# Feature 128 of two neighbouring slices on two groups of 32 rows of the array, their two small products issued together

## The reference

```python
def _attn_ref(x):                       # x: 2 x 3008 x 256
    X = np.fft.fft(x, axis=1)
    X = np.fft.fft(X, axis=2)
    return X.real.astype(np.float32)

def _moe_ref(x, w_in, w_out):           # w_in 256 x 2048, w_out 2048 x 256
    h = x @ w_in
    g = np.where(h > 0.0, h, 1.0 * (np.exp(np.minimum(h, 0.0)) - 1.0))
    return (g @ w_out).astype(np.float32)

def _moe2_ref(x, w_in, w_out, alpha):   # the same shapes, alpha 2048
    h = x @ w_in
    g = np.maximum(h, 0.0) + alpha * np.minimum(h, 0.0)
    return (g @ w_out).astype(np.float32)
```

## Time and profile before

| | |
|---|---|
| median of 3 runs | 984.11 us (982.59 to 984.53) |
| the profiled execution's own time | 983.52 us |
| its span, first to last instruction | 981.7 us |
| outside the span | 1.8 us |
| TensorE busy (matmuls) | 964.7 us, 98%, 4466 matmuls |
| TensorE busy (weight loads) | 800.9 us, 82% |
| VectorE busy | 784.3 us, 80% |
| ScalarE busy | 621.1 us, 63% |
| GpSimd busy | 165.3 us, 17% |
| granted TensorE clock | 1.000 |

### The profile page before, as it was taken

One profiled execution on the slowest core, in us unless ns is written; L12 is line 12 of the kernel. 1 busy time (PEld: TensorE's weight loads), 2 busy tenths in 40 slices (PEclk: granted clock), 3 DMA queues, 4 the chain that ended last, 5 costly groups with the idle time before them and its releaser, 6 DMA issues.

```text
span 981.7 us, 12208 instructions
## 1 busy us (share of the span) xinstructions
PE 964.7 (98%) x4466; PEld 800.9 (82%) x4466; DVE 784.3 (80%) x879; ACT 621.1 (63%) x808; POOL 165.3 (17%) x186
## 2 busy tenths in 40 slices
PE   7999999999999999999999999999999999999997
PEld 5877888888888888888888888888888888888886
DVE  3369997897887998889788788788878878877765
ACT  2358887887887787777755556555555555655453
POOL 3357431231321651017100000000000000000000
PEclk9999999999999999999999999999999999999999
DMA  8501030210211345321310110011011011000101
GB/s 235 161 22 55 1 140 1 97 43 1 97 44 75 108 165 208 153 90 72 108 38 1 44 44 0 1 44 43 1 44 43 0 38 44 1 1 1 43 1 43
DMA packets 11031, 57.69 MB, mean 59 GB/s; under 512 B 1706, under 2 KB 2410, under 8 KB 7388
## 3 DMA queue, kind: packets, MB, share of 16 engines
q1 hardware_dynamic: 6188, 28.44, 8.3%
q0 software_dynamic: 4784, 28.48, 8.1%
HBM read 32.88 MB, written 24.01 MB: 58 GB/s over the span
## 4 chain that ended last, share of the span: by engine, by line
PE 58%; DVE 2%; issue 0%; ACT 0%; DVEq 0%; ACTq 0%
PE ACC L581 9%; PE ACC L583 9%; PE ACC L582 9%; PE PQ L533 8%; PE PQ L535 8%; PE PQ L534 8%; PE ACC L551 2%; PE ACC L556 2%; PE ACC L552 2%; DVE Gl L865 1%; PE PQ L514 0%; PE PQ L515 0%; PE PQ L516 0%; PE PQ L520 0%; PE PQ L519 0%
## 5 line engine op out<-in xcount | busy, mean ns | idle before, releaser
L551 PE MATMUL ACC<-Gh,W 128*128 128x512 f32 x372 | 144.9, 389 | 2.5 <-DVE Gl L865 2.4
L552 PE MATMUL ACC<-Gl,W 128*128 128x512 f32 x372 | 143.7, 386 | 0.0
L865 DVE SCALAR_TENSOR_TENSOR Gl<-G,Gh 128x1024 fp32r<-128x1024 f32 (+1 forms) x96 | 121.9, 1270 | 26.9 <-ACT Gh L687 26.2
L867 DVE TENSOR_TENSOR Gl<-G,Gh 128x1024 fp32r<-128x1024 f32 (+1 forms) x96 | 115.2, 1200 | 17.4 <-ACT Gh L689 17.0
L842 DVE SCALAR_TENSOR_TENSOR G<-H,G 128x1024 f32<-128x1024 f32 (+1 forms) x96 | 126.8, 1321 | 0.6 <-ACT G L708 0.6
L581 PE MATMUL ACC<-Gh,W 128*128 128x512 f32 x324 | 124.8, 385 | 2.1 <-DVE Gl L867 2.1
L689 ACT ACTIVATE Gh<-G 128x1024 fp32r<-128x1024 f32 (+1 forms) x96 | 100.3, 1045 | 39.6 <-DVE G L857 34.7
L583 PE MATMUL ACC<-Gh,W 128*128 128x512 f32 x324 | 124.5, 384 | 0.0
L582 PE MATMUL ACC<-Gl,W 128*128 128x512 f32 x324 | 124.5, 384 | 0.0
L857 DVE SCALAR_TENSOR_TENSOR G<-H,G 128x1024 f32<-128x1024 f32 (+1 forms) x96 | 115.5, 1203 | 3.3
L556 PE MATMUL ACC<-Gh,W 128*128 128x512 f32 x372 | 113.4, 386 | 0.0
(11 more groups left out here) (116 smaller groups left out, 1795.9 us busy)
## 6 DMA issues: line engine op xcount, KB each, us to landing
w_scratch<-stage POOLq DMA_DIRECT2D x4, 1792.0 KB, 7.2
xr<-in_x SPq DMA_DIRECT2D x16, 384.0 KB, 4.0
raw<-in_w POOLq DMA_DIRECT2D x24, 256.0 KB, 4.5
W3a<-w_scratch POOLq DMA_DIRECT2D x3, 1792.0 KB, 12.0
y_scratch<-y_st SPq DMA_DIRECT2D x5, 1024.0 KB, 3.9
y_in<-y_scratch SPq DMA_DIRECT2D x5, 1024.0 KB, 4.8
out_y<-y_st SPq DMA_DIRECT2D x5, 1024.0 KB, 3.9
w_scratch<-stage POOLq DMA_DIRECT2D x4, 1024.0 KB, 4.9
```

The source lines that it names most:

```text
L551: mm(o, W2[:, f, 0, sl], Gh[:, j, c:c + w], start=f == 0, stop=False)
L552: mm(o, W2[:, f, 0, sl], Gl[:, j, c:c + w], start=False, stop=False)
L865: stt(Gl[:, j, 0:n], G[:, j, 0:n], bias, f32(Gh[:, j, 0:n]), ALU.add, ALU.subtract).then_inc(lo_ready, 1)
```

## The change

`W1e` and `eo(t, 4)` now hold the three parts of feature 128 on partitions 0, 1, 2 (for even slices) and once more on 32, 33, 34 (for odd ones). The small product of a slice takes only its group of 32 partitions. The small products of slice s (odd) and s + 1 are issued one right after the other at the end of `up1(s)`. The second of them opens the sum in its PSUM bank (`start=True`), which the other three matmuls of `up1(s + 1)` then add to. The small products of slices 0 and 95 stay alone. The wait for `combine(s - 1)` moves with the pair from the head of `up1(s + 1)` to the end of `up1(s)`; the wait at the head stays too. `up_done` of an even slice is signalled by L520's matmul. `move_row` and `load_e` issue six DMAs each in place of three. `FLIP_AT` of tiles 1 to 4 goes from 8 to 9, as the PQ buffer of an even slice is in use by then.

```diff
-FLIP_AT = (3, 8, 8, 8, 8)
+FLIP_AT = (3, 9, 9, 9, 9)
+ER = 32
             def load_e(t):
-                for p, part in ((0, 0), (PT // 4, 0), (PT // 2, 1)):
-                    src = e_dram[part:part + 1, NQ * t:NQ * (t + 1), :].rearrange("o q k -> o (q k)")
-                    sp.dma_start(f32(eo(t, 4)[p:p + 1, :]), src).then_inc(e_in[t % 2], 16)
+                for group in range(2):
+                    for p, part in enumerate((0, 0, 1)):
+                        src = e_dram[part:part + 1, NQ * t:NQ * (t + 1), :].rearrange("o q k -> o (q k)")
+                        sp.dma_start(f32(eo(t, 4)[ER * group + p:ER * group + p + 1, :]), src).then_inc(e_in[t % 2], 16)
...
             def move_row(n, a, b):
-                for p, part in ((0, 2), (32, 3), (64, 2)):
-                    row = f32(W1e[p:p + 1, :]).rearrange("p (f c) -> p f c", f=NF)[:, a:b, :]
-                    gp.dma_start(row, f32(W1[0:1, a:b, part, :])).then_inc(w1e_in, 16)
-                gp.wait_ge(w1e_in, 48 * (n + 1))
+                for p, part in enumerate((2, 3, 2)):
+                    for group in range(2):
+                        row = f32(W1e[ER * group + p:ER * group + p + 1, :]).rearrange("p (f c) -> p f c", f=NF)
+                        gp.dma_start(row[:, a + group:b:2, :], f32(W1[0:1, a + group:b:2, part, :])).then_inc(w1e_in, 16)
+                gp.wait_ge(w1e_in, 96 * (n + 1))
...
+            def extra(s, start):
+                t, f = s // NF, s % NF
+                group = slice(ER * (f % 2), ER * (f % 2) + ER)
+                return mm(PQ[:, f % 2, 0:TW], W1e[group, f * PT:(f + 1) * PT], eo(t, 4)[group, :], start=start, stop=not start)
...
                 if f == 0:
                     pe.wait_ge(eol_ready, t + 1)
-                    pe.wait_ge(e_in[t % 2], 48 * (t // 2 + 1))
+                    if t == 0:
+                        pe.wait_ge(e_in[0], 96)
...
                 o = PQ[:, j, 0:TW]
-                mm(o, W1[:, f, 0, :], eo(t, 0), start=True, stop=False)
+                mm(o, W1[:, f, 0, :], eo(t, 0), start=s == 0 or j == 1, stop=False)
                 mm(o, W1[:, f, 0, :], eo(t, 2), start=False, stop=False)
-                mm(o, W1[:, f, 1, :], eo(t, 0), start=False, stop=False)
-                mm(o, W1e[:, f * PT:(f + 1) * PT], eo(t, 4), start=False, stop=True).then_inc(up_done, 1)
+                ins = mm(o, W1[:, f, 1, :], eo(t, 0), start=False, stop=s > 0 and j == 0)
+                if s == 0:
+                    ins = extra(s, False)
+                if j == 1 and s + 1 < S1:
+                    pe.wait_ge(comb_ready, s)
+                    if s + 1 == LATE_F:
+                        pe.wait_ge(w1_ready, 2)
+                    if f == NF - 1:
+                        pe.wait_ge(e_in[(t + 1) % 2], 96 * ((t + 1) // 2 + 1))
+                    ins = extra(s, False)
+                    extra(s + 1, True)
+                elif j == 1:
+                    ins = extra(s, False)
+                ins.then_inc(up_done, 1)
```

## The result

The changed kernel takes 992.47 us in the median of four runs (991.26 to 994.05), the one before 983.94 us in the same comparison. The ratio is 1.0092, with a 95% interval of 1.0079 to 1.0105: slower by 0.9%, or 8.5 us. The forecast was 991.5.

The account below looks back on a forecast made before the run. TensorE's dense matmul stream was taken as the bound. Net +0.15 us a pair (0.32 + 0.055 - 0.227) gave +7.0 for 47 pairs, +0.64 for slices 0 and 95, +0.1 for moved waits: +7.8, put at 991.5 us, range 980 to 998.

Parts of the forecast that it names:

- The bound and the covers: TensorE's dense stream sets the time: 0.227 us per matmul, holes cost full length; other engines' work and DMAs stay covered.
- the cover for the DMAs: Three more DMAs in move_row and first load_e: 6 us of cover before TensorE starts at 56.38, so they cost nothing.
- The moved wait: Wait for combine now before the pair: covered by 2.1 us in steady state, uncovered in slice 1; put at +0.1 us.
- The price of two changes: Going from 128 to 32 rows and back around each pair: 0.32 us for hole and open load, bounds 0 and 0.38.
- The second product's load: Weight load of a pair's second small product delays it by 0.055 us, half of 0.11; bounds 0 and 0.11.
- rival P: In each pair the second product is wholly free, the changes are paid: +5.1 us, 988.6 us; chance 0.20.
- The sign that I had named: TensorE timeline: two rounds of up1 and down1, 8.62 us before, take 8.77 under A and 8.40 under F.
- A: The forecast itself, at the pairs: changes cost 0.32 us, the second load shows in part; 991.5 us, chance 0.40.
- The other sign: From odd slice's L520 to L551 behind the pair: 0.83 us under A, 0.77 under P, 0.45 under F, 1.0 under S.
- F: Faster: changing from 128 to 32 rows at the pairs makes no hole, loads keep their lead; -10.6 us, 973; chance 0.15.
- H: Half the price at the pairs: only the hole or the open load, 0.16 us for two changes; -2.8 us, 980.7; chance 0.12.
- S: The pair doesn't overlap: with changes paid +15.7 us, 999, chance 0.08; without them 983.5, chance 0.05.

## Why the prediction was right, and where it was off

**The bound and the covers held.** Each matmul's worth of 0.227 us, the full price of a hole in the stream, and the cover for the DMAs came out as put (4.08 us for 18 slots, waits of 2.3 us, up1 at 56.36). The moved wait cost under the 0.1 us that I gave it.

**The price of two changes was the mis-sized term: 0.42 measured, 0.32 put.** It was above the 0.38 that I had called its upper bound. I had taken the hole at 0.08 and the open load at 0.08 for each way. The hole in front of the pair is 0.09 and the open load behind it 0.10 and a little more, as the earlier trace rows have them for the L444 matmuls; the largest part of what I took too low is the pair's own slot, 0.20 for its load and its end, where I had 0.16 by the smaller of the values (0.05 for 46 columns of weights, 0.06 for the small matmul before the way back). The product has 128 columns of weights and 512 of stream, so the larger rows were the nearer ones. Of the missing 0.10, this slot holds 0.04, the hole in front and the load behind 0.03, and the matmuls after them, for which I had put nothing, 0.03. That prices read off matmuls of 64 and 128 columns can be carried to 512 was taken for granted, and holds: the half width shows the same 0.20 for 256 and 512. The Trainium skill's rule, that changing the tiling mode drains TensorE ("TensorEngine Tiling (Array Packing)", Key Properties), agrees with the trace: the load that stood a matmul ahead (202.40 for 202.62) stands at its matmul (95.93 for 95.94).

**The second product's load was put at 0.055, and is 0.** Here rival P was right: four loads start within 0.01 us. The 0.11 that I had halved is the distance of loads to the same rows, which the run with one group shows (0.29 for two loads in place of 0.18). The Trainium skill ("TensorE: Matmul & The Clock Gate", Part 3) says that a weight load overlaps matmuls in flight only where the two take different groups of rows, and the trace agrees in that loads to two or four groups start together and two to one group don't.

**The two errors nearly cancelled.** 0.42 - 0.227 = +0.195 a pair where 0.32 + 0.055 - 0.227 = +0.15 was put: 9.2 us in place of 7.0. Slices 0 and 95 add 0.8. To these 10 us the order adds 1.3, and yet the first layer grew by 9.05 only: the waits that a slower round hides took back 2.2, a term that was missing in the sum. So that the total came out within 1 us of the 991.5 is in part luck: the trip was put 4.7 us too low over the 47 pairs and the second product 2.6 too high, and the order's cost and the hidden waits, both left out but for 0.1, nearly cancelled as well. The sign that I had named, two rounds of 8.77 us under A, came out at 8.81, at the upper end of A (the load at 0.11) by its total, and for another reason: P's free second product with a dearer trip. The other sign misleads in the same way: from the last full matmul to the `down1` behind the pair, open load counted in, are 96.36 - 95.62 + 0.10 = 0.84 us, where A had 0.83 and P 0.77.

**The rivals.** F falls with every load that has lost its lead, and H with the 0.42, which holds both the hole and the open loads. S falls with the run on one group, which is what S looks like: 4.95 us for a pair's round in place of 4.73. That its 999.4 us meets the 999 put for S is luck again, as the trip costs 0.42 and not 0.32 and the waits hid some of it. For F I had counted that `row128` changes its columns as well. The worry had no ground: here the pair keeps all 128 columns and the hole is there, and with 64 columns over full rows there is none. What makes the one between L468 and L469, where the rows stay at 64, is open.

## What to carry to other kernels

Before splitting a product over groups of rows, look how often the stream must go from full rows to few and back. In a dense stream like this one (fp32r, 512 columns, full clock), set 0.42 us a trip against 0.227 us for each product that is saved: two a trip lose, four win. Put as many small products into one trip as there are groups and free PSUM banks, and don't make the trip for one or two. In a stream without waits, the record to look at is the weight load: where it has lost its lead on its matmul, TensorE has stood still, though its busy share says 98%.

## What the runs showed of the hardware

- Going to 32 rows and back costs 0.42 us for one product or two, for 256 columns or 512, and 0.03 to 0.05 more for four products. With two products on groups of 64 rows it costs the same 0.42.
- Up to four products of 32 rows on four groups, into four PSUM banks, run side by side, loads included: 0.42 us for two, 0.43 for four.
- Two on the same group run one after the other: 0.24 us more from load to load, 0.22 by the rounds.
- Weights of 64 columns in place of 128, over full rows, make no such hole (0.02 us a round). What the one between L468 and L469 in the earlier trace rows is, isn't shown.
- A price on the bound engine isn't wholly paid where its waits lie: 96 x 0.42 = 41 us were put in, 35.5 came out.
